# Logits from the turn of the attention output, routing batch by batch, and a last stage in sorted order

## The reference

```
scores = q @ k.T / sqrt(64)                      # batch 4, 8 heads, 576 rows, head size 64
scores = where(scores >= max - tau, scores, -1e9); attn = exp(scores - max)
x = (attn / (sum + 1e-9)) @ v                    # tokens 2304 x 512
logits = x/(|x|+1e-6) @ (emb/(|emb|+1e-6)).T / tau2
e = argmax(logits); gate = softmax(logits)[e]    # 8 experts
y = gate * (relu(x @ w1[e]) @ w2[e])             # 512 -> 1024 -> 512
h = y @ w_in; out = (max(h,0) + alpha*min(h,0)) @ w_out    # 512 -> 2048 -> 512
```

## Time and profile before

| | |
|---|---|
| median of 3 runs | 1128.76 us (1127.71 to 1129.24) |
| the profiled execution, own time | 1130.75 us |
| its span, first to last instruction | 1129.1 us |
| TensorE busy (PE) | 1035.6 us, 92% |
| VectorE busy (DVE) | 570.9 us, 51% |
| ScalarE busy (ACT) | 454.3 us, 40% |
| GpSimd busy (POOL) | 327.9 us, 29% |

### The profile page before, as it was taken

How to read it: one execution, slowest core, us unless ns; L and a number is a source line. 1 busy time by engine, 2 the same in 40 slices (tenths; PEclk the granted TensorE clock), 3 DMA queues, 4 the chain that set the end, 5 groups by cost and what they waited for, 6 DMA issues and landing times.

```text
span 1129.1 us, 20591 instructions
## 1 busy us (share of the span) xinstructions
PE 1035.6 (92%) x6751; PEld 903.6 (80%) x6752; DVE 570.9 (51%) x1176; ACT 454.3 (40%) x875; POOL 327.9 (29%) x423
## 2 busy tenths in 40 slices
PE   3999999999999914999999998799999999999997
PEld 3888888888888713888888886799999999898996
DVE  4888888888888331212222222554444444444442
ACT  3777777777777551222222222421212122122111
POOL 1133333311111546669976824210100001000000
PEclk8999999999999956999999999799999999999999
DMA  6435444443342234345545424500001000000001
GB/s 175 97 79 137 105 121 114 124 114 83 92 112 78 59 138 168 112 135 209 195 158 185 166 70 156 168 29 28 28 1 38 20 28 28 0 28 0 28 1 28
DMA packets 135675, 102.66 MB, mean 91 GB/s; under 512 B 107964, under 2 KB 107980, under 8 KB 135124
## 3 DMA queue, kind: packets, MB, share of 16 engines
q1 hardware_dynamic: 124548, 74.36, 22.7%
q0 software_dynamic: 4752, 16.26, 4.1%
q10 hardware_dynamic: 6336, 11.54, 3.0%
HBM read 78.01 MB, written 24.12 MB: 90 GB/s over the span
## 4 chain that ended last, share of the span: by engine, by line
PE 83%; DVE 6%; issue 5%; ACT 3%; SPq 1%; DMA 1%; DVEq 0%; POOL 0%; ACTq 0%
PE bank L604 70%; PE bank L607 13%; DVE q_st L1207 2%; ACT square L1040 1%; DVE neg_max L1178 1%; SPq L373 1%; DVE kl_st L1217 1%; ACT kh_st L958 1%; ACT exps L939 0%; DVE x_tail_sb L1235 0%; DVE x_tail_sb L1234 0%; DVE X L1228 0%; DMA y_got<-y_sorted,pos 0%; DVE probs L1189 0%; DVEq L1228 0%
## 5 line engine op out<-in xcount | busy, mean ns | idle before, releaser
L604 PE MATMUL bank<-x_hi,ring 128*128 128x384 f32 x768 | 212.4, 340 | 1.5 <-DVE x_lo L1422 1.5
L604 PE MATMUL bank<-ring,g_hi 128*128 128x512 f32 x576 | 179.2, 392 | 0.0
L1128 ACT ACTIVATE g_hi<-act 128x384 fp32r<-128x384 f32 x96 | 50.5, 526 | 300.5 <-DVE act L1438 300.5
L604 PEld LDWEIGHTS bank<-x_hi,ring 128*128 128x128 f32 x768 | 141.2, 189 | 4.8 <-issue 1.9
L514 POOL TENSOR_TENSOR ring<-stage,ring 128x2048 fp32r<-128x2048 f32 x31 | 142.6, 4600 | 4.6
L1435 DVE TENSOR_SCALAR neg<-bank,alpha_col 128x384 f32<-128x384 f32 x96 | 59.2, 617 | 150.5 <-PE bank L604 150.5
L604 PE MATMUL bank<-x_lo,ring 128*128 128x384 f32 x384 | 129.9, 338 | 0.0
L1189 DVE SCALAR_TENSOR_TENSOR probs<-bank,thresh,exps 128x576 f32<-128x576 f32 x144 | 117.3, 815 | 23.3 <-ACT exps L939 14.0
L604 PEld LDWEIGHTS bank<-ring,g_hi 128*128 128x128 f32 x576 | 107.0, 188 | 18.1
L1178 DVE TENSOR_REDUCE neg_max<-bank 128x1 f32<-128x576 f32 x144 | 108.3, 752 | 19.1 <-PE bank L604 16.9
L939 ACT ACTIVATE exps<-bank,neg_max 128x576 f32<-128x576 f32 x144 | 106.8, 742 | 22.1 <-DVE neg_max L1178 20.4
(11 more groups left out here) (171 smaller groups left out, 1625.7 us busy)
## 6 DMA issues: line engine op xcount, KB each, us to landing
stage<-in_moe_w SPq DMA_DIRECT2D x32, 1024.0 KB, 5.1
qraw<-in_q SPq DMA_DIRECT2D x68, 128.0 KB, 2.8
kraw<-in_k SPq DMA_DIRECT2D x68, 128.0 KB, 3.0
x_sorted<-X POOLq DMA_DIRECT2D x13, 512.0 KB, 4.1
x_row<-x_sorted ACTq DMA_DIRECT2D x23, 256.0 KB, 2.7
y_sorted<-y_row ACTq DMA_DIRECT2D x21, 256.0 KB, 2.2
vraw<-in_v SPq DMA_DIRECT2D x32, 128.0 KB, 2.7
stage<-in_moe_w_in SPq DMA_DIRECT2D x4, 1024.0 KB, 4.9
```

Source lines behind the costliest of these rows:

```text
L604: return nc.tensor.matmul(dst, lhsT, rhs, start=start, stop=stop)
L1128: nc.scalar.activation(g_hi[f % 3][:, :], act2[f % 2][:, :], ACT.Copy).then_inc(g_hi_ready, 1)
```

## The change

The expert vectors stand beside the identity in a tile `turner`, divided by the temperature, so that the matmul that turns an attention output gives the logits of its two heads in 16 more columns. The turn is then a float matmul by `turner`, no longer a transpose. `normalise` scales these columns into `part_logit`. After each batch VectorE adds them over heads, finds the expert and the rank of each token in eleven small steps, spread over units (`route_step`); TensorE adds the ranks (`rank`), POOL scatters the batch's tiles. Each expert has a fixed region of CAP rows in `x_sorted`, so positions don't wait for the counts of later batches. A row of X now carries 16 more numbers: its eight logits and its place in the output. The rest behind the last unit is the ranking of batch 3, of the last tile, the tables, and zeros behind each expert's rows. The pairs' loops are written out straight.

In the expert stage ScalarE takes the sum of squares of each slot, and y is stored without padding, row after row, with its squares, logits and place. The last stage takes tiles in sorted order with plain loads, so that turns need no gate; the gates are computed in VectorE's and ScalarE's gaps in the first group and applied where `o_row` is copied; POOL scatters `o_row` to its place. All of w_in is split by POOL.

```diff
-        outT = at("outT", [P, P])
+        outT = [at(f"outT{i}", [P, P]) for i in range(2)]
+        turner = at("turner", [P, DC, TURNED])  # P + 2 * EXPERTS columns
+ROUTES = ((0, 4), (4, 4), (8, 5), (13, 4), (17, 1))  # first tile, number of tiles
+        def out_bank(n, j):
+            return {3: S_BANK[1], 4: S_BANK[0]}.get(j, M_BANK) if n == PAIRS - 1 else M_BANK
+        def route_unit(g, k):
+            return unit_after(4 * g + 4, 2, k)
...
@@ SP
             def store_tail(n):
+                t, at_p = TAIL_TILES[n // 8], TAIL * (n // 4 % 2)
                 for h in range(2):
-                    sp.dma_start(dst, x_tail_sb[h * TAIL:(h + 1) * TAIL, :]).then_inc(tail_stored, 16)
+                    sp.dma_start(X[at_p:at_p + TAIL, ...], x_tail_sb[rows, 0:HEAD]).then_inc(tail_stored, 16)
+                    sp.dma_start(part_logit[at_p:at_p + TAIL, at_l:at_l + EXPERTS],
+                                 x_tail_sb[rows, HEAD:HEAD + EXPERTS]).then_inc(tail_stored, 16)
...
@@ POOL
             for n in range(PAIRS):
                 small_steps(n)
-                if 1 <= n <= ZERO_PAIRS:
-                    pool.dma_start(x_slots[:, 2 * n - 2:2 * n, :], zeroes...).then_inc(zero_stored, 16)
+                # in small_steps, behind part(n, j): four or five units from route_unit(g, 10)
+                            if (n, j) == route_unit(g, 10 + k):
+                                pool.wait_ge(pos_ready, g + 1)
+                                scatter(ROUTES[g][0] + k)
...
-            split_pieces(1, 1, 0, 4)
-            for t in range(TT):
-                pool.indirect_dma_start(x_sorted, IndirectOffsetOnAxis(ap=pos[:, t:t + 1], axis=0), ...)
-            split_pieces(1, 1, 4, PIECES)
+            for g in (3, 4):
+                pool.wait_ge(pos_ready, g + 1)
+                for t in range(ROUTES[g][0], sum(ROUTES[g])):
+                    scatter(t)
+            for e in range(EXPERTS):
+                pool.indirect_dma_start(x_sorted, IndirectOffsetOnAxis(ap=zero_pos[:, e:e + 1], axis=0),
+                                        zero_row[:, :], None).then_inc(zeroed[min(e, 2)], 16)
+            pool.dma_start(x_sorted[EXPERTS * CAP:EXPERTS * CAP + 2 * P, :]..., zero_row...).then_inc(zeroed[2], 16)
+            split_pieces(1, 1, 0, PIECES)
...
-            pool.wait_ge(y_stored, end * 16)
-            for t in range(TT):
-                pool.indirect_dma_start(y_got[t % GT][:, :], None, y_sorted, IndirectOffsetOnAxis(ap=pos[:, t:t + 1], axis=0))
+            pool.wait_ge(y_stored, but_one * 32)
+            for t in range(GT):
+                load_y(t)
+            pool.wait_ge(y_stored, all_slots * 32)
+            pool.dma_start(meta[:, :, :], y_sorted[0:TOKENS, D:YC]...).then_inc(meta_in, 16)
...
+                    pool.wait_ge(o_ready, t + 1)
+                    pool.indirect_dma_start(out, IndirectOffsetOnAxis(ap=rows[:, t, META:META + 1], axis=0), o_row[tt][:, :], None)
@@ PE
+            def rank(g):
+                pe.wait_ge(hot_ready, g + 1)
+                first = mm(dst, tri[:, :], hot[:, :, 1:nt + 1], True, False)
+                mm(dst, ones[:, :], cum[:, :, 0:nt], False, True).then_inc(rank_done, 1)
...
-                turn(bank[:, M_BANK, P:2 * P], outT[:, :]).then_inc(out_turned, 1)
+                mm(bank[:, out_bank(n, j), P:P + TURNED], outT[(UNITS * n + j) % 2][:, :], turner[:, n % 4, :], True, True)\
+                    .then_inc(out_turned, 1)
...
-            turn_x(0)
-            for g in range(ROUTE_GROUPS): ...              # turns, logits, folds
+            rank(3)
+            rank(4)
@@ ACT
+                    if s == 0:
+                        square_slot(i + 1)                 # behind the first Relu
             def store_y(i):
+                row = act.value_load(slot_row[0:1, ds(i, 1)], ...); at_y = act.value_load(slot_pos[0:1, ds(i, 1)], ...)
                 act.wait_ge(y_ready, i + 1)
-                act.dma_start(y_sorted[ds(i * P, P), :], y_row[:, :]).then_inc(y_stored, 16)
+                act.dma_start(y_sorted[ds(at_y, P), 0:D + 1], y_row[:, :]).then_inc(y_stored, 16)
+                act.dma_start(y_sorted[ds(at_y, P), D + 1:YC], x_sorted[ds(row, P), D:D + META]).then_inc(y_stored, 16)
...
+            act.wait_ge(scattered, 16 * TT)
+            act.wait_ge(zeroed[0], 16)
+            act.dma_start(x_row[:, :], x_sorted[ds(row, P), :]).then_inc(xs_in, 16)
+            act.wait_ge(zeroed[2], 16 * (EXPERTS - 1))     # before for_slots
...
-            for tt in range(GT):
-                gate_tile(tt)
+            act.wait_ge(slots_done, end)
             for tt in range(GT):
                 split_tile(0, 0, tt)
...
-                    nc.scalar.activation(o_row[tt][:, :], bank[:, 2 + tt, :], ACT.Copy).then_inc(o_ready, 1)
+                    nc.scalar.activation(o_row[tt][:, :], bank[:, 2 + tt, :], ACT.Copy, scale=gate[:, t:t + 1]).then_inc(o_ready, 1)
@@ DVE
+                    V.tensor_tensor(part_logit[:, at_l:at_l + 2 * EXPERTS]..., got_l..., row_inv[:, j, :]..., ALU.mult)
                     V.tensor_tensor(X[:, at_x:at_x + P]..., got..., row_inv[:, j, :]..., ALU.mult).then_inc(x_ready, 1)
...
+                for h in range(2):
+                    V.tensor_scalar(x_tail_sb[rows, 0:HEAD], got[rows, ...], row_inv[rows, j, 0:1], None, ALU.mult)
+                    last = V.tensor_scalar(x_tail_sb[rows, HEAD:HEAD + EXPERTS], got_l[rows, ...], row_inv[rows, j, 0:1], None, ALU.mult)
...
+            def route_step(g, k):
+                # 0 sum over heads, 1 max, 2 is_ge, 3 mult, 4 min, 5 is_equal, 6 scan -> hot_ready,
+                # 7 rank * hot (waits rank_done), 8 sum, 9 cast -> pos_ready, 10 carry to the next group
...
             normalise(PAIRS - 1, UNITS - 2)
+            for k in range(7):
+                route_step(3, k)
             normalise(PAIRS - 1, UNITS - 1)
+            route_step(3, 10)
+            for k in (7, 8, 9):
+                route_step(3, k)
+            for k in range(10):
+                route_step(4, k)
...
-                V.tensor_copy(y_row[:, :], bank[:, 5, :]).then_inc(y_ready, 1)
+                dve.wait_ge(squared, i + 1)
+                V.tensor_copy(y_row[:, D:D + 1], ssq_slot[:, ds(i, 1)])
+                V.tensor_copy(y_row[:, 0:D], bank[:, 5, :]).then_inc(y_ready, 1)
```

More of the change, by code:

```diff
@@ L46 @@
 MIN_SLOTS = TOKENS // P
+TABLE = 32
+CAP = TOKENS + P
+META = EXPERTS + 1
+XC = D + 16
+YC = D + 1 + META
 WCHUNK = 1024
@@ L151, in build @@
         emb_n = at("emb_n", [EXPERTS, 4])
+        alpha_row = at("alpha_row", [F2C, P])
+        x_tail_sb = at("x_tail_sb", [P, HEAD + EXPERTS])
+        part_logit = at("part_logit", [P, TT * HEADS * EXPERTS])
+        r_hot = [at(f"r_hot{i}", [P, EXPERTS * 6]) for i in range(2)]
+        r_cum = [at(f"r_cum{i}", [P, EXPERTS * 6]) for i in range(2)]
+        r_keep = {nt: at(f"r_keep{nt}", [P, EXPERTS * (nt + 1)]) for nt in (1, 4, 5)}
+        r_best, r_first, r_pos = (at("r_" + n, [P, 5]) for n in ("best", "first", "pos"))
@@ L157, in build @@
[L157 to L172, removed]
+        zero_row = at("zero_row", [P, XC])
+        place[0] = work_at + 4 * CHUNKS * 2 * HEAD
+        cnt, slots, slots_in, row_step, pos_step = (at("s_" + n, [1, EXPERTS]) for n in ("cnt", "slots", "in", "row", "pos"))
@@ L257, in build @@
         pos_ready = sem("pos_ready")
+        zero_ready = sem("zero_ready")
+        zeroed = [sem(f"zeroed{i}") for i in range(3)]
         scattered = sem("scattered")
@@ new lines, in _ @@
+            pool.wait_ge(meta_in, 16)
+            rows = meta[:, :, :].bitcast(U32)
+            for g in range(GROUPS):
+                if g + 2 < GROUPS:
+                    for tt in range(GT):
+                        pool.wait_ge(x2_turned, (g + 1) * GT + tt + 1)
+                        load_y((g + 2) * GT + tt)
+                for tt in range(GT):
+                    t = g * GT + tt
+                    pool.wait_ge(o_ready, t + 1)
+                    pool.indirect_dma_start(out, IndirectOffsetOnAxis(ap=rows[:, t, META:META + 1], axis=0),
+                                            o_row[tt][:, :], None).then_inc(o_stored[tt], 16)
@@ L601, in _ @@
+            for tt in range(GT):
+                pool.wait_ge(o_stored[tt], 16 * GROUPS)
         @block.tensor
@@ L1006, in _ @@
                 split(1, 1, g, FIRST_BANKS[g])
-            for_pairs(act, pair)
+            for n in range(PAIRS):
+                pair(n, n % 2, n // 2)
             copy_rest(PAIRS - 1, UNITS - 1, 1)
@@ L1282, in _ @@
                 split(1, 1, g, FIRST_BANKS[g])
-            for_pairs(dve, pair)
+            V.tensor_copy(iota_i[:, :], iota_int[0:1, :])
+            V.tensor_scalar(iota_k[:, :], iota_int[0:1, 0:TT], float(P), None, ALU.mult)
+            V.tensor_copy(iota_p[:, :], iota_pint[:, :])
+            V.tensor_scalar(base_e[:, :], iota_int[:, 0:EXPERTS], float(CAP), None, ALU.mult)
```

(7 more changed lines are left out.)

693 lines of the change are left out of this document (348 added, 345 removed).

## The result

The new kernel takes 1101.0 us in the median (1100.25 to 1101.79, 4 runs) beside 1128.24 us (1127.52 to 1129.24) for the kernel before: a ratio of 0.9758, 95% interval 0.9741 to 0.9775. The forecast was 1106.0 us, with a range of 1093 to 1124. The profiled execution has a span of 1098.5 us and an own time of 1100.25.

A forecast was written before the change was run, and what follows sets the result against it. TensorE was taken to bound the expert and last stages, VectorE and TensorE the attention chain. 1.0 + 17 + 5.5 - 38.6 - 8.3 + 0.8 = -22.6 us gave 1106.2 us, range 1093 to 1124.

The forecast's parts named there:

- a turn: Attention: float matmul of 144 columns costs 0.15 us more per turn; two of five per pair on TensorE's chain, 0.3 us.
- The units: Attention: VectorE's new 128x16 multiply from PSUM in four units, 0.1 us each, three on the chain, 0.3 us per pair.
- the tail: Attention: two more 64x8 multiplies by a column per pair, 0.22 us each, 0.44 us ahead of TensorE's awaited row.
- Ranking: Attention: three batches ranked by VectorE steps, rank matmuls and POOL scatters, together +5.5 us, bounds 3 and 9.
- rival 4: Attention: the gaps take most of the additions, total 1096 us; chance 0.13.
- Routing: Last attention turn to first expert matmul: first matmul at 400.6 instead of 439.19, -38.6 us.
- they keep their length unless a new wait opens: Expert and last stages: TensorE is busy throughout and no edit takes a matmul from either, so no change.
- Rivals 1 and 2: Expert stage: small VectorE copy blocked by POOL's splits, at random (+13 us, 0.17) or in step (up to +53, 0.05).
- 1.5 us of lateness being free: Expert stage: with the second y store, 1.5 us of lateness is free; anything over stalls TensorE.
- Hand-over: Last expert matmul to last stage: first matmul at 706.5 instead of 714.81, -8.3 us, bounds -10 and -5.
- rival 5: Hand-over stays long because loads or loop exits are late, total 1114 us; chance 0.07.
- The end: Three o_rows stored by POOL scatters 1.27 us apart instead of SP stores: +0.8 us, bounds 0 and 2.5.

The follow-up runs named there:

- b1: Kernel before, with each attention output turned by a float matmul of 144 columns instead of a transpose: 1128.41 us beside 1128.96 (0.9997).
- b2: b1 plus VectorE scaling the 16 columns in the four units and twice 8 columns in the tail unit: 1136.72 us (1.0072).
- c2: New kernel with expert tiles moved, tail logits stored first, first late tiles loaded early, SyncE waiting for last scatters, x2 at multiple of 128 bytes: 1097.13 us (0.9717).
- b3: New kernel with one more VectorE copy of 128x18 per slot, SBUF to SBUF, ahead of the copy of one number: 1106.21 us.
- a4: New kernel with the last three output tiles stored by SyncE as plain stores instead of GpSimd's scatters: 1094.26 us (0.9689).
- a2: New kernel with the expert stage's tiles from xT_hi on moved by 448 bytes: 1094.63 us (0.9698).
- b4: New kernel with xT tiles at a multiple of 128 bytes, hT tiles 64 beyond, x2 tiles 32 beyond: own time 1100.78 us, one execution.
- c1: New kernel, unchanged, run again: 1101.82 us (0.9754).

## Why the prediction was right, point by point

The direction and its cause, a shorter routing, were right, and the time came out 5.0 us below the forecast. The terms of the sum, against the measured change from trace to trace (both columns against the profiled executions):

| term | predicted | measured |
|---|---|---|
| start, to the first maximum | +1.0 | +1.3 |
| turns, multiplies, ranking in the attention | +17 + 5.5 | +7.2 |
| last masking to first expert matmul | -38.6 | -37.9 |
| expert stage | 0 | +4.0 |
| hand-over | -8.3 | -7.4 |
| last stage | 0 | -3.9 |
| end | +0.8 | +6.2 |
| sum | -22.6 | -30.5 |

The medians differ by only 27.2 us, as the profiled execution of the kernel before was 2.5 us above the median of 1128.24 (the prediction took 2.0, from 1128.76), and that of the new kernel 0.75 us below its own. That the total came within 5 us is in part luck: the attention was 15.3 us cheaper than forecast, the end 5.4 us dearer, and two changes of 4 us that were not forecast cancel.

**The step that was mis-sized is the attention**, by 15.3 us. I priced a turn at 0.15 us more, two of them on the chain, and b1 measured nothing for all five: they add 0.07 us each to TensorE's busy time, and its gaps take that. Which gaps was not tried. The units were priced at 0.3 us per pair and cost 0.15, the tail at 0.44 and cost 0.29. Ranking was priced at 5.5 us as if VectorE had no gap; it cost 1 to 2.4, by the two counts above. The bounds given, +8 to +33 for the units, left the 6.75 us of b2 just outside: rival 4, at 1096, was right for this term.

**Routing** was right to 0.7 us, partly by luck. From the last turn to the first expert matmul I had 20.3 us and the trace has 22.3, 2 us too few; but the stretch from the last masking to the last turn, which I took as it was, shrank from 5.95 to 4.58 us. The last tile's ranking began 7.2 us after the last turn instead of 5.6, as the last of four stores landed 2.59 us after its issue; the load of x_row waited for the tables and not for the zero scatter. In c2, issuing logits first and waiting for one table alone brought 1.7 us together. Its chain then runs over GpSimd's scatters and the landing of the first zero scatter (2.73 us), the path that I had predicted; as that was only 0.2 to 0.3 us behind the tables, nearly all of the 1.7 us must come from the stores. The two were not tried apart.

**The expert stage** was taken as fixed because TensorE is full and no matmul was added. The step that failed is "they keep their length unless a new wait opens": TensorE can be full and slower. Rivals 1 and 2 are refuted, as the small copy takes 0.15 us; b3 shows that their mechanism exists for a wider one. Their price rested on 1.5 us of lateness being free; b3 has 0.65 us, and in the new kernel the second y store's issue ends at 501.77 and the next Relu starts at 502.25, 0.48 us later. With a blocked copy both rivals would have been dearer than I said. **The last stage** failed in the same step with the other sign. These two errors cancel (+4.0 and -3.9), and the total does not show them.

**Hand-over** (-7.4 for -8.3, rival 5 not needed) and the square at no cost were right. **The end** was mis-sized: I counted issues 1.27 us apart, 0.8 in all, and not what follows the last landing. a4 puts the scatters of the last group, with GpSimd's wait for them, at 7.4 us.

## What to carry to other kernels

A stage in which TensorE is always busy is not of fixed length: if a tile grows, look at where the tiles behind it now start, and compare the pace of one kind of matmul in both traces, before any wait is suspected. Price small additions by the gaps of the whole period, not by the duration of each row, and expect a saved wait to come back at the next instruction that stands too early in program order. The last transfers of a kernel should not be GpSimd's scatters, if something else can store them.

## What the runs showed of the hardware

- The pace of 512-column fp32r matmuls depends on the place of the stationary tile in its partition: three in 0.68 or 0.69 us when it starts at a multiple of 128 bytes, 0.70 us at 64 beyond (a2, b4, c1). That is 2 to 3% of the time of such matmuls, 5 us of 265. Other places were not tried, and why is open.
- It depends on another tile's place too. With the x2 tiles at 32, 96, 128 and 160 bytes beyond a multiple of 512, nine `project` matmuls took 2.08, 2.04, 2.08 and 2.04 us, and twelve `hidden` ones 2.08, 2.08, 2.11 and 2.12 (before, after, c2, b4). x2 is not read by `project`. No rule follows from four places, and why is open; places have to be tried.
- A copy of 128x18 between SBUF tiles waited for a running GpSimd split to end (up to 1.43 us instead of 0.17, b3), one of 128x1 never did (0.15 us in all 21 slots, a split running in 16 of them, after). Widths between were not tried.
- With GpSimd's scatters last, the span ended 6.2 us after the last packet to the output, and 3.9 us after it when SyncE did the waiting (after, c2). With SyncE's stores last it ended 0.8 us after it (before: 1128.25 and 1129.06).
